# Fused attention and two MoE layers: in the last pair of heads, nine output steps of the first head with each of four tiles, and the second head's output from the ninth tile on

## The reference

```
q_pool = q.reshape(B, H, S // 2, 2, D).mean(axis=3)      # 576 queries
scores = scale * np.matmul(q_pool, k.transpose(0, 1, 3, 2))   # 576 x 1152
attn = np.exp(scores - np.max(scores, axis=-1, keepdims=True))
attn = attn / (np.sum(attn, axis=-1, keepdims=True) + 1e-09)
x = np.matmul(attn, v)                                   # per head 576 x 64
x = (sigmoid(x @ w_gate) * (x @ w_val)) @ w_out          # 1152 tokens, 512 -> 1536 -> 512
for e in range(8):                                       # router weights P from 8 Sinkhorn rounds
    out += P[:, e:e + 1] * (np.maximum(x @ w1[e], 0.0) @ w2[e])
```

## Time and profile before

| what | value |
|---|---|
| time, median of 3 runs | 1239.49 us (1237.88 to 1241.13) |
| the profiled execution: its time, its span | 1238.6 us, 1236.8 us |
| PE busy | 1226.6 us, 99% of the span |
| DVE, ACT, POOL busy | 790.3, 585.9, 645.7 us |
| granted TensorE clock, mean | 1.000 |
| scores of the last pair's tile 4 to the transposes of its last tile | 233.94 to 253.71 us |

### The profile page before, as it was taken

The page is one execution under the profiler, slowest core; times in us unless marked ns, Lnnn a source line. Parts: engine busy times, 40 slices in busy tenths (PEclk is TensorE's granted clock), DMA queues, the critical chain, the costliest instruction groups (busy, mean ns, idle before and its releaser), DMA issues.

```text
span 1236.8 us, 19909 instructions
## 1 busy us (share of the span) xinstructions
PE 1226.6 (99%) x7613; PEld 1132.0 (92%) x7613; DVE 790.3 (64%) x1694; ACT 585.9 (47%) x1228; POOL 645.7 (52%) x525
## 2 busy tenths in 40 slices
PE   8999999999999999999999999999999999999999
PEld 7998989999999899989999999998998998998998
DVE  7998999986863145775475375375376476466444
ACT  7999999944433244444353243243243243233221
POOL 6688888738962475554254264254254254254220
PEclk9999999999999999999999999999999999999999
DMA  6777777501121431221221221221221222222112
GB/s 169 120 121 121 121 121 120 96 18 34 52 70 34 125 98 35 78 77 51 69 86 52 68 85 52 69 86 51 69 81 56 69 72 66 69 69 69 52 34 94
DMA packets 98831, 95.25 MB, mean 77 GB/s; under 512 B 14512, under 2 KB 73200, under 8 KB 98736
## 3 DMA queue, kind: packets, MB, share of 16 engines
q1 hardware_dynamic: 98416, 93.63, 30.9%
q10 hardware_dynamic: 320, 0.34, 0.1%
HBM read 88.47 MB, written 2.40 MB: 73 GB/s over the span
## 4 chain that ended last, share of the span: by engine, by line
PE 89%; ACT 5%; POOL 2%; issue 2%; DMA 1%; DVE 0%; SPq 0%; POOLq 0%; DVEq 0%
PE bank L1291 14%; PE bank L1293 13%; PE bank L1292 13%; PE bank L1545 11%; PE bank L1546 11%; PE bank L1547 11%; PE bank L1171 3%; PE bank L1144 3%; PE bank L1184 2%; ACT probs L1659 2%; PE bank L1257 2%; PE bank L1259 2%; PE bank L1258 2%; PE bank L1185 2%; ACT pT_hi L1573 2%
## 5 line engine op out<-in xcount | busy, mean ns | idle before, releaser
L2253 DVE TENSOR_TENSOR c<-bank,c 128x256 f32<-128x256 f32 (+1 forms) x448 | 197.3, 457 | 281.4 <-PE bank L1293 274.8
L1072 POOL TENSOR_TENSOR w_lo<-w_raw,w_hi 128x512 fp32r<-128x512 f32 x128 | 163.7, 1300 | 287.7 <-ACT w_hi L1573 287.7
L1546 PE MATMUL bank<-w_lo,h_hi 128*128 128x512 f32 x578 | 225.2, 390 | 0.0
L1545 PE MATMUL bank<-w_hi,h_hi 128*128 128x512 f32 x578 | 225.1, 390 | 0.0
L1547 PE MATMUL bank<-w_hi,h_lo 128*128 128x512 f32 x578 | 224.4, 388 | 0.0
L1865 ACT ACTIVATE h_hi<-c 128x256 fp32r<-128x256 f32 (+1 forms) x256 | 112.5, 445 | 160.3 <-DVE c L2253 160.0
L1547 PEld LDWEIGHTS bank<-w_hi,h_lo 128*128 128x128 f32 x578 | 108.5, 188 | 22.9
L1573 ACT ACTIVATE c<-bank 128x256 f32<-128x256 f32 (+1 forms) x64 | 26.3, 410 | 214.7 <-PE bank L1293 214.7
L1545 PEld LDWEIGHTS bank<-w_hi,h_hi 128*128 128x128 f32 x578 | 108.6, 188 | 20.8
L1546 PEld LDWEIGHTS bank<-w_lo,h_hi 128*128 128x128 f32 x578 | 108.6, 188 | 20.1
L2018 DVE TENSOR_REDUCE part_min<-bank 128x1 f32<-128x288 f32 (+2 forms) x216 | 108.8, 552 | 21.4 <-PE bank L1185 19.4
(11 more groups left out here) (210 smaller groups left out, 3140.4 us busy)
## 6 DMA issues: line engine op xcount, KB each, us to landing
w_raw<-in_moe_w SPq DMA_DIRECT2D x64, 512.0 KB, 3.6
w_raw<-in_moe_w SPq DMA_DIRECT2D x64, 256.0 KB, 3.1
q_raw<-in_q SPq DMA_DIRECT2D x30, 288.0 KB, 4.7
k_raw<-in_k SPq DMA_DIRECT2D x30, 288.0 KB
wo_raw<-in_moe_w_out SPq DMA_DIRECT2D x16, 384.0 KB, 3.3
v_raw<-in_v SPq DMA_DIRECT2D x16, 288.0 KB, 4.6
gv_raw<-in_moe_w_gate SPq DMA_DIRECT2D x12, 256.0 KB, 3.0
gv_raw<-in_moe_w_val SPq DMA_DIRECT2D x12, 256.0 KB, 3.6
```

The costliest lines, as they stand in the source:

```text
L1072: ins = nc.gpsimd.tensor_tensor(w2_lo[:, u % 2, c], w2_raw[:, c], f32(w2_hi[:, u % 2, c]), ALU.subtract)
L1545: nc.tensor.matmul(dst, hh, wh, start=(first and c == 0), stop=False)
L1546: nc.tensor.matmul(dst, hh, wl, start=False, stop=False)
L2253: nc.vector.tensor_tensor(dst[:, 0:w], bank[:, (u + b) % 3, 0:w], other[:, 0:w], ALU.add).then_inc(done, 1)
```

## The change

LAST_AV_STEPS is a second table for the pair that begins with head 14. The 36 steps of head 14 go nine each with tiles 4 to 7 and none with tile 8, so that head 15's steps follow right behind tile 8's transposes. ACT's copy of head 14's second half stands one tile earlier (tile 7 for 8); its copy of the first half stays at tile 6. DVE takes piece 2 of tile g = 69 between the second and the third minimum of tile 8, no longer behind nmax.

```diff
 AV_STEPS = (9, 9, 9, 9, 6, 6, 6, 9, 9)
+
+LAST_AV_STEPS = (9, 9, 9, 9, 9, 9, 9, 9, 0)
@@
                 if i >= COMMON:
-                    for n in range(sum(AV_STEPS[COMMON:i]), sum(AV_STEPS[COMMON:i + 1])):
+                    steps = LAST_AV_STEPS if h_last(2 * pair) else AV_STEPS
+                    for n in range(sum(steps[COMMON:i]), sum(steps[COMMON:i + 1])):
                         av(2 * pair, n)
@@
                 if i == 6:
                     o_out(h, 0, 0)
-                if i == 8:
+                if i == (7 if h_last(h) else 8):
                     o_out(h, 0, 1)
@@
                 for j in range(NKB):
+
+                    if h == NHEAD - 1 and i == 8 and j == 2:
+                        p_lo(g - 2, 2)
                     dve.wait_ge(s_ready, 3 * g + j + 1)
@@
-                if g >= 2:
+                if g >= 2 and not (h == NHEAD - 1 and i == 8):
                     p_lo(g - 2, 2)
```

## The result

The changed kernel takes 1244.29 us (median of 21) against 1240.13 for the kernel before (21), ratio 1.0033 with a 95% interval of 1.0023 to 1.0043: some 4.2 us slower. Here and in all experiments, executions in a slower state that comes whatever the kernel (one each of e2, e4 and the kernel before, 1334 to 2455 us) are left out of every median, ratio and count. The profiled execution of the changed kernel took 1245.07 us.

The account below looks back on a forecast made before the run. PE was taken to bound the kernel. A 2.97 us pause plus 0.10 in tile 8, less 0.40 in each of tiles 4, 5 and 6 and 0.13 in tile 7, gave 1.74; forecast 1241.3 us, range 1239.3 to 1244.0.

Parts of the forecast that it names:

- What bounds the kernel; handed on to the end: PE, busy 1226.6 of 1236.8 us, is the bound; what it loses or wins in attention reaches the end unchanged.
- Three more steps in tiles 4 and 5 are free: The added steps, 0.40 us per tile, fit PE's waits for ACT; six steps done early win 0.80 us.
- Tile 6, the wait moves forward: Step 18, now first in tile 6, waits for ACT's second copy; PE stands still for 2.97 us.
- Tiles 7 and 8, the sum: Tile 7 takes 3.23 us, not 3.37; tile 8 has a 0.10 us wait; all terms sum to 1.74 us later.
- The tail becomes the bound: Rival: tile 8's later exponentials or piece 2 of g = 70 hold g = 71's transposes; 2.5 us, 1242.0, chance 0.05.
- The tie: Piece 2 of tile g = 70 ends at 256.46; PE needs it at 256.51 for g = 71's last four transposes.
- Does a still PE lose its clock?: Rival: half pace behind tile 6's pause loses 2.4 us more, 4.2 in all, 1243.7 us; chance 0.11.

Follow-up runs that it names:

- e2: The changed kernel with 18 idle transposes on PE in the pause ahead of step 18; 1240.03 against 1238.62 us for the kernel before, ratio 1.0010.
- e4: The changed kernel without the moved piece (DVE's piece 2 behind nmax again); 1243.09 against 1238.62 us for the kernel before, ratio 1.0034.
- e5: The changed kernel unedited, timed and profiled again as a control; 1241.59 against 1238.11 us for the kernel before, ratio 1.0027.
- e1: The changed kernel with ACT's two first-half copies in tile 5, its gv_hi copy in tile 6; 1237.49 against 1238.62 us before, ratio 0.9989.
- e6: The changed kernel with ACT's two copies earlier within tile 6, ahead of piece 2's high part; 1240.50 against 1238.11 us before, ratio 1.0018.
- e3: The kernel before with head 14's last-pair steps 9, 9, 0, 9, 9 for tiles 4 to 8; 1238.63 against 1238.62 us, ratio 1.0004.
- e8: The kernel of e1 without the moved piece (DVE's piece 2 behind nmax); 1238.13 against 1238.11 us for the kernel before, ratio 0.9998.
- e7: The kernel of e1 with DVE's sum of head 14's first rows behind pieces 0 and 1 of g = 71; 1237.39 against 1238.11 us before, ratio 0.9992.

## Why the prediction was wrong

The measured 1244.29 us lie outside the range, by 0.3 us. The rise was 4.2 us, and 3.5 in e5, against 1.8 forecast. Step by step:

- *What bounds the kernel; handed on to the end*: right. The spans of the two profiles differ by 6.5 us, and 2.95 before tile 4 with 3.50 from there to the transposes of g = 71 make all of it. Only the 3.50 are the change's.
- *Three more steps in tiles 4 and 5 are free*: right. From tile 4's first score to tile 6's transposes it is 8.62 us in e5 (233.38 to 242.00) and was 8.61 (233.94 to 242.55).
- *Tile 6, the wait moves forward*: right. Forecast as 2.97 us from readiness to start; the transposes of tile 6 to step 18 are 3.96 us (242.00 to 245.96 in e5), 0.90 of them the transposes' own, so 3.06. The 0.09 on top are the signal: in e5 the copies end at 245.00 + 0.81 = 245.81 and step 18 starts 0.15 later, where 0.06 was assumed (first row below).
- *Tiles 7 and 8, the sum*: right where the clock held. The sum was 1.74 us; e5's and e2's profiles show 1.89 and 1.89, and the executions of e5 at full clock are 1.8 us slower. The 0.15 between are the signals: 0.09 at step 18, and at head 15's first step a wait of 0.17 (251.52 to 252.59 is 1.07, 0.90 of them transposes) for the 0.10 forecast, since PE starts 0.14 behind the end of DVE's piece (251.77 + 0.68 = 252.45). Tile 7 took 3.24 (248.28 to 251.52), as forecast. From e5's timelines of ACT, DVE and PE:

```profile
245.00 0.81 ACT L1576 ACTIVATE o_all<-bank 64x288 f32<-64x288 f32 x2
...
251.77 0.68 DVE L1960 TENSOR_TENSOR pT_lo<-bank,pT_hi 128x512 fp32r<-128x512 f32 x1
...
252.59 0.37 PE L1173 MATMUL bank<-pT_hi,v_st 128*128 128x288 f32 x1
```

- *The tail becomes the bound*: it did not in the changed kernel, where the last four transposes stand 1.07 us behind the first five (1.06 before). The tie that the prediction saw there, 256.46 against 256.51, counts the moved piece twice: the 2.94 us behind nmax hold its 0.59 (250.15 to 250.74), which the change takes out. Without it piece 2 of tile g = 70 ends at 255.87, in time by 0.6. In e1 and in e6 the tail did hold PE, through DVE's sum of rows, which the prediction had at its old length of 0.44 us and which took 1.33 and 1.85.
- *Does a still PE lose its clock?* This step failed. The mechanism was there, with a price of 2.4 us and a total of 4.2 us; its chance was put at 0.11, so the forecast's sum had no term for it. The mean clock was under 1.000 in 25 of 32 executions. The reason given against it was that no row of the trace shows the pace fall behind a pause. But no row shows a pause over 0.97 us in work (the 1.67 us stand ahead of PE's first instruction, and the pace behind them was half), so the trace had nothing to say, and its silence was taken for a no. One fall measured 1.7 us, less than the 2.4 that the pace at the kernel's start had given; that with 1.74 us of order the prediction's price came to 4.2, as the medians did, is in part luck. The Trainium skill (TensorE: Matmul & The Clock Gate, What's actually happening) has the slow clock as the default, which activity releases. The measured clock agrees, 0.50 from 252 to 254 us; whether a pause of this length was enough only the runs could say.

## What to carry to other kernels

When a step with a wait is moved ahead, move what it waits for as well: here two copies of 0.41 us each, one tile later than needed, turned a change worth about 1 us of gain (e1: 0.8 in the trace, 1.4 by the ratio) into 1.8 us of loss, and the clock into some 4. A new pause like those here (2.34 and 2.82 us) on a TensorE that was nearly always busy must be priced with half clock behind it, though the trace before shows no such fall; a trace without long pauses is no evidence on them. Transposes that nobody uses, put into the pause and into a free bank, tell within one run whether a loss is the pause or the clock (e2).

## What the runs showed of the hardware

- The clock fell while PE was busy again, about 1.1 us after a pause of 2.82 us had ended (249.48 to 250.62), and stayed at half for some 3.4 us. With the same pause it did not fall in e5's profiled execution.
- A DVE sum of two SBUF operands (64x288, 0.44 us alone) that starts under a GpSimd instruction ended 0.30 to 0.32 us behind it in four profiles (e1, e3, e6, e8). From e3's timelines of DVE and POOL:

```profile
250.23 2.65 DVE L1987 TENSOR_TENSOR o_all<-o_all 64x288 f32<-64x288 f32 x1
...
250.16 2.40 POOL L922 TENSOR_TENSOR gv_lo<-gv_raw,gv_hi 128x1024 fp32r<-128x1024 f32 x1
```

The sum ends at 252.88, 0.32 behind 252.56. In e1 it is 251.75 behind 251.43, the same 0.32; moved out from under GpSimd, in e7, it took 0.44. In the kernel before it took 0.44 too: it started at 250.74, as one GpSimd instruction ended (250.75), and the next, x_lo, took 1.60 us where it has 1.41 to 1.43 in the other profiles. The Trainium skill (SBUF — State Buffer, Who interferes with whom) says that a DVE instruction with two SBUF inputs contends with one of GpSimd that reads SBUF, that the shared ports are an exclusive lock, and that the order of issue decides who blocks; the rows agree.
